# A block's turn and routing logits moved from its first step into its second, ahead of a long hook

## The reference

```
# 1. linear attention with decay: 4 batches, 8 heads, 768 steps, head size 48
cur = einsum(u * k_t, v_t);  y_t = einsum(r_t, state + cur);  state = w * state + einsum(k_t, v_t)
# 2. dense gated layer, d_ff 1536
x = (silu(y @ w_gate) * (y @ w_val)) @ w_out
# 3. mixture of experts: 8 experts, top 1, d_ff 1024
logits = x @ w_gate2; e = argmax(logits); gate = softmax(logits)[e]
eom = 1 / (1 + exp(-(x @ w_output_gate)))
out = gate * eom[e] * (relu(x @ w1[e]) @ w2[e])
```

## Time and profile before

| | |
|---|---|
| median of the runs | 833.06 us (832.24 to 833.59) |
| the profiled execution's own time | 832.38 us |
| its span, first to last instruction | 830.5 us (1.9 us lie around it) |
| TensorE busy, by the profile | 816.4 us, 98% |
| VectorE, ScalarE, GpSimd busy | 58%, 44%, 23% |
| mean granted TensorE clock | 0.998 |

### The profile page before, as it was taken

How to read it: one execution, slowest core, us unless ns; L and a number is a source line. 1 busy time by engine, 2 the same in 40 slices (tenths; PEclk the granted TensorE clock), 3 DMA queues, 4 the chain that set the end, 5 groups by cost and what they waited for, 6 DMA issues and landing times.

```text
span 830.5 us, 19906 instructions
## 1 busy us (share of the span) xinstructions
PE 816.4 (98%) x7813; PEld 719.6 (87%) x7813; DVE 479.3 (58%) x1004; ACT 368.3 (44%) x705; POOL 189.8 (23%) x159
## 2 busy tenths in 40 slices
PE   7999999999999999999999999999999999999996
PEld 4788888888888888888888888899999999999996
DVE  7667743445443535344343453469878977897771
ACT  3635432333323333223332311456566866687661
POOL 3434402322352143404220210004021110111010
PEclk9999999999999999999999999999999999999999
DMA  9445301121211113121100116057997667866700
GB/s 338 160 172 181 118 1 62 62 86 40 97 62 62 39 63 121 63 61 40 63 25 1 40 40 266 2 229 239 353 364 282 246 249 279 303 254 234 286 19 19
DMA packets 24148, 116.72 MB, mean 141 GB/s; under 512 B 3373, under 2 KB 9825, under 8 KB 18449
## 3 DMA queue, kind: packets, MB, share of 16 engines
q1 hardware_dynamic: 19984, 101.16, 33.8%
q0 software_dynamic: 3520, 9.87, 3.1%
q10 hardware_dynamic: 576, 4.72, 1.6%
HBM read 102.64 MB, written 14.16 MB: 141 GB/s over the span
## 4 chain that ended last, share of the span: by engine, by line
PE 98%; DMA 0%; DVE 0%; issue 0%; POOLq 0%; ACT 0%; SPq 0%
PE bank L1775 36%; PE bank L1823 7%; PE bank L1825 6%; PE bank L1824 6%; PE bank L1896 5%; PE bank L1898 5%; PE bank L1897 5%; PE bank L1861 3%; PE bank L1863 3%; PE bank L1862 3%; PE bank L1857 3%; PE bank L1700 2%; PE bank L1650 2%; PE bank L1685 1%; PE bank L1837 1%; PE bank L1858 1%
## 5 line engine op out<-in xcount | busy, mean ns | idle before, releaser
L1355 DVE TENSOR_TENSOR PP<-SG,bank 128x512 f32<-128x512 f32 (+1 forms) x78 | 49.9, 646 | 209.7 <-PE bank L1775 178.0
L1775 PE MATMUL bank<-X1H,WH 128*128 128x512 f32 x432 | 168.7, 391 | 0.0
L1775 PE MATMUL bank<-X1L,WH 128*128 128x512 f32 x432 | 168.0, 390 | 0.2 <-DVE X1L L1179 0.2
L1775 PE MATMUL bank<-X1H,WL 128*128 128x512 f32 x432 | 168.0, 390 | 0.0
L793 ACT ACTIVATE AH<-PP 128x512 fp32r<-128x512 f32 (+1 forms) x78 | 46.0, 597 | 152.7 <-DVE PP L1355 152.7
L897 ACT ACTIVATE SG<-bank 128x512 f32<-128x512 f32 x72 | 43.0, 597 | 158.5 <-PE bank L1775 152.9
L1775 PEld LDWEIGHTS bank<-X1H,WH 128*128 128x128 f32 x432 | 81.0, 188 | 17.9 <-issue 1.0
L1775 PEld LDWEIGHTS bank<-X1H,WL 128*128 128x128 f32 x432 | 81.0, 188 | 17.2 <-DVE WL L1173 0.3
L1775 PEld LDWEIGHTS bank<-X1L,WH 128*128 128x128 f32 x432 | 81.0, 188 | 17.0 <-DVE X1L L1179 0.6
L1823 PE MATMUL bank<-AH,WH 128*128 128x512 f32 (+1 forms) x234 | 91.0, 389 | 0.0
L776 POOL DMA_INDIRECT out<-YO,IDX x31 | 38.5, 1241 | 218.0 <-ACT YO L991 208.5
(11 more groups left out here) (245 smaller groups left out, 1799.7 us busy)
## 6 DMA issues: line engine op xcount, KB each, us to landing
W_EVEN<-w SPq DMA_DIRECT2D x20, 1536.0 KB, 9.1
W_ODD<-w SPq DMA_DIRECT2D x18, 1536.0 KB, 8.7
RK_IN<-unit_rk SPq DMA_DIRECT2D x19, 736.0 KB, 5.3
V_IN<-unit_v SPq DMA_DIRECT2D x20, 480.0 KB, 3.6
STG<-w_dense ACTq DMA_DIRECT2D x4, 1152.0 KB, 5.2
XG_ODD<-store SPq DMA_DIRECT2D x9, 394.0 KB, 8.4
store<-PAD SPq DMA_DIRECT2D x8, 394.0 KB
STG<-w_dense SPq DMA_DIRECT2D x2, 1152.0 KB, 9.4
```

What stands on the lines that cost most here:

```text
L1355: return tt(PP[:, part], SG[:, part], VALUE_PS[:, part], ALU.mult)
L1775: last = mm(bank_[:, :], lhs[:, f, m, k * P:k * P + P], rhs[:, k, :], start=(x == 0), stop=(x == len(terms) - 1))
```

## The change

In blocks 1 to 5 the turn of the rows and the routing logits move from the hook of step 0 to that of step 1. In blocks 1 to 4 the units' hooks move one step earlier, from steps 2, 4, 6, 8 to steps 1, 3, 5, 7, so that turn and logits stand directly ahead of the first long hook. The logits no longer go to the value's bank but to bank 7, columns 384 to 511, beside the scores; so the waits for the value's bank around them go (`value_free` ahead of the logits, `logits_copied` ahead of the value's `up` in step 1), and the scores of a unit now wait for `logits_copied`. The copies that follow the turn and the logits on ScalarE and VectorE move to step 1 as well. In the last block, which has no units, everything of the routing stands one step later: turn and logits in step 1, turned logits in step 2, ranks and positions in step 3. Block 0 keeps its order.

```
     def unit_begun(n, f):
         final = isinstance(n, int) and n >= CH - 2
-        if f in (2, 4, 6) and not (final and n == CH - 1):
+        if isinstance(n, int) and n == 0 and f in (0, 2, 4, 6):
             return units_of_block(n)[f // 2]
-        if f == 0 and isinstance(n, int) and n == 0:
-            return units_of_block(n)[0]
-        if f == 8 and not final:
+        if not (isinstance(n, int) and n in (0, CH - 1)) and f in (1, 3, 5):
+            return units_of_block(n)[f // 2 + 1]
+        if f == (8 if isinstance(n, int) and n == 0 else 7) and not final:
             return units_of_block(n + 1)[0]
         return None
...
-                self.logits = (ps if isinstance(n, int) and n == CH else VALUE_PS)[:, 0:P]
+                self.logits = ps[:, 2 * PART:2 * PART + P]
...
# ScalarE
+                    if f == 1 and not first:
+                        rec_copies(n)
                     begun, ended = unit_begun(n, f), unit_ended(n, f)
...
-                    if f == 0 and not first:
-                        rec_copies(n)
...
# VectorE
-                        if f == 0:
+                        if f == 1:
                             copy_logits(n)
-                        if f == (1 if last else 9):
+                            rec_copy(n)
+                        if f == (2 if last else 9):
                             copy_turned_logits(n)
-                        if f == (2 if last else 10):
+                        if f == (3 if last else 10):
                             copy_ranks(n)
...
-                        if f == 0:
-                            rec_copy(n)
-                        if f == (1 if last else 9):
+                        if f == (2 if last else 9):
                             route(n)
-                        if f == (2 if last else 10):
+                        if f == (3 if last else 10):
                             positions(n)
...
# TensorE
-                    if f == 1 and not first:
-                        pe.wait_ge(logits_copied, n)
...
-                        if f == 0:
+                        if f == 1:
                             turn(n)
-                            pe.wait_ge(value_free, q + 1)
+                            need(pe, ranks_copied, n - 1)
                             route_logits(n)
-                        if f == (1 if last else 9):
+                        if f == (2 if last else 9):
...
-                        if f == (2 if last else 10):
+                        if f == (3 if last else 10):
                             ranks(n)
...
                     if begun:
                         if not begun.in_block_0:
                             pe.wait_ge(silu_ready, q + 1)
+                            need(pe, logits_copied, n)
                             need(pe, ranks_copied, max(n - 1, 0))
                         scores(begun)
```

More of the change, by code:

```diff
@@ L349, in unit_summed @@
     def unit_summed(n, f):
-        if f in (2, 4, 6, 8) and not (isinstance(n, int) and n >= CH - 2):
-            return units_of_block(n)[f // 2 - 1]
+        if isinstance(n, int) and n == 0:
+            return units_of_block(n)[f // 2 - 1] if f in (2, 4, 6, 8) else None
+        if f in (1, 3, 5, 7) and not (isinstance(n, int) and n >= CH - 2):
+            return units_of_block(n)[f // 2]
         return None
     def unit_ended(n, f):
[L357 to L360, removed]
+        if f in (1, 3, 5, 7) and not (isinstance(n, int) and n == CH - 1):
+            return units_of_block(n)[f // 2]
         return None
@@ L1921, in dense_block @@
                     if not first:
-                        if f == 0:
+                        if f == 1:
                             turn(n)
-                            pe.wait_ge(value_free, q + 1)
+                            need(pe, ranks_copied, n - 1)
                             route_logits(n)
-                        if f == (1 if last else 9):
-                            if begun:
-                                pe.wait_ge(parts_masked, 2 * (begun.i - BATCH) + 2)
+                        if f == (2 if last else 9):
+                            if not last and n < CH - 2:
+                                pe.wait_ge(parts_masked, 2 * (units_of_block(n + 1)[0].i - BATCH) + 2)
                             turn_logits(n)
-                        if f == (2 if last else 10):
+                        if f == (3 if last else 10):
                             ranks(n)
```

## The result

| | before | after |
|---|---|---|
| median of 18 runs each, us | 832.78 | 835.77 |
| lowest to highest, us | 831.67 to 834.36 | 834.61 to 841.51 |
| ratio, 95% interval | | 1.0043 (1.0034 to 1.0052) |
| profiled execution, us | 832.38 | 834.61 |
| its span, us | 830.5 | 832.8 |

The change makes the kernel slower, by 0.34% to 0.52%. The forecast was 832.4 us with a range up to 833.6: the sign and the range were both wrong. The profiled execution of after is the fastest of its runs, so what follows accounts for 2.2 us; for the 1.2 us by which the median lies above it no execution was profiled.

What follows compares the result with a forecast made beforehand. TensorE, busy in 98% of the span, was taken as the bound. Four blocks' merge gain of 0.88 us less 0.2 for the new neighbourhood, all else nothing, gave -0.7: 833.06 to 832.4 us, range 831.1 to 833.6.

Steps and rivals of the forecast that it cites:

- Plain steps and the merge: TensorE, blocks 1 to 4: two hooks become one, ups of steps 0 to 2 fall from 12.50 to 12.28 us.
- The charge for the switch: TensorE, blocks 1 to 4: state terms or outputs directly behind the logits cost 0.05 us each, 0.2 us in all.
- The wait that comes. … Cost nothing: Scores of the first long hook wait for `logits_copied`; the copy comes 1.6 us ahead of need, so no cost.
- Last block. … Zero: Last block: turn and logits go from step 0 to 1, hook entry and exit both still paid; no change in time.
- The other half of that step: Last block, VectorE: step 4's product comes 1.5 us late, with 1.5 us of cover, so nobody waits.
- GpSimd: Blocks 2 to 4: RW ready 3.3 us ahead of second unit's scores; rival: late, 839.0 us at most, chance 0.07 with other waits.
- The clock: Dense hooks keep granted clock at 1.00; rival: level lost for a step in four blocks, 24 us, 857, chance 0.01.

Runs made afterwards that it cites:

- e9: After with the last block's turn and logits back in step 0, two repeated score waits dropped, 136 spare waits in block 0: 830.47 us, ratio 0.9983.
- e7: Before with 64 long-met spare waits among the matmuls of block 0's ups, nothing else changed: 835.28 us, ratio 1.0028 to before.
- e8: Before with 128 long-met spare waits among the matmuls of block 0's ups, nothing else changed: 836.44 us, ratio 1.0045 to before.
- e4: After with 128 long-met spare waits among the matmuls of block 0's ups: 834.20 us, ratio 1.0019 to before.
- e6: After with the last block's turn and logits back in step 0, two repeated score waits dropped, 128 spare waits in block 0: 833.39 us, ratio 1.0003.
- e1: After without the scores' repeated waits TensorE had already passed, a spare wait in the following down instead: 835.40 us, ratio 1.0043 to before.
- e2: After with the last block's turn and logits, and what follows them, back in step 0 as in before: 834.60 us, ratio 1.0033 to before.
- e5: After with the last block's turn and logits back in step 0, two repeated score waits dropped, no spare waits: 835.99 us, ratio 1.0030 to before.
- e10: After with the last block's turn and logits back in step 0, two repeated score waits dropped, 212 spare waits in block 0: 832.66 us, ratio 1.0001.
- e11: After with 133 spare waits, its seventh wait and last block left as they are: 833.29 us, ratio 1.0010 to before.

## Why the prediction was wrong

**Plain steps and the merge: right.** 0.22 us a block, as read from the starts. The charge for the switch, 0.05 a block, should have been a gain of 0.11 in blocks 1 to 3. Together e9 against before gives 427.27 - 0.38 - 425.55 = 1.3 us, where 0.7 was forecast and 0.9 the end of the range kept.

**"The wait that comes. … Cost nothing": the step that failed first.** The copy was in time in nine of ten profiles of the new order, as the cover of 1.6 us said. But the wait itself is a part of an instruction of TensorE's, and it stands in every hook with scores, not only in the first one of a block, since the line of the diff is under every unit. In eleven hooks it is the seventh wait and made the fourth semaphore instruction, 0.10 us, 1.1 us in all. Before showed three such instructions at this place; their number and spacing could have been read.

**"Last block. … Zero": failed.** I had carried "the `down` waits for the copies, which end earlier, nothing" from the middle blocks. There 2.9 us of units lie between logits and `down`; in the last block nothing does, and VectorE's copy of the rows, which stands behind its low part and the logits' copy, ends at 480.15, while the `down` could have begun at 479.12. It begins 1.1 us late. The prediction had VectorE's copies as the later ones, and that held. The cover was worked out for one place and used at another. The other half of that step was right: VectorE's product of step 4 begins at 500.77 where the earlier trace rows has 497.29, which is 1.3 us late beside a block that is 2.2 us later, and TensorE waits for nobody there:

```profile
500.77 0.69 DVE L1355 TENSOR_TENSOR PP<-SG,bank 128x512 f32<-128x512 f32 x1
```

**No term for where the instruction pieces end: the largest miss.** A hook that moves a step earlier also moves its instructions by some hundred places in TensorE's stream. Neither sum nor rivals had it. The rows of before that would have hinted at it were there: scores of 1.06 us at 134.03, and a column of instruction packets. It could hardly have been given a sign, only a width. Before has next to no stops by luck, as its shifts show; these versions of one and the same kernel (before, e7, e8) differ by up to 0.45%, 3.7 us, and my whole range was 2.5 us wide.

**GpSimd: right in the likely case.** After the change RW of block 2's second unit ends 3.49 us ahead of its scores, against 3.3 worked out:

```profile
206.31 1.15 POOL L709 TENSOR_TENSOR KH<-RK_IN,POWT 128x448 f32<-128x448 f32 x1 [2.42 <-DMA store<-RC,POSI]
...
211.34 1.28 POOL L704 TENSOR_TENSOR RW_ODD<-RK_IN,POWR 112x512 f32<-112x512 f32 x1
```

**The clock** is at 1.00 in the middle block (203.71 to 293.20), as the earlier trace rows had let expect of dense hooks. It falls behind a long stop (e4, e6), which the hooks themselves don't make.

**What stays open.** Stops come at fixed remainders, but their length does not follow from the place: instruction 7617 cost 0.83 us in after, 1.52 in e1, 0.91 in e2, and nothing in before. It follows from the packet, which took 0.93, 1.32 and 0.92 us in the three; in before it had landed 3.75 us ahead. Why a packet begins late and takes 0.88 to 1.45 us is open. The spread of after's runs (6.9 us against 2.7) fits stops of changing length and the clock behind a long one; no run was profiled at 841.51 to show it. The waits for `XG_ODD` in e5 to e8, and for `HL` in e4, e10 and e11 (0.83 to 1.07 us), are not explained.

## What to carry to other kernels

A wait costs its own instruction even if it is long met: on a queue that is 98% busy count the waits, in every pass that the edited line serves, and drop those the engine has already passed. Work out the cover of a move at each place where the order differs, the last pass above all. And where an engine runs through hundreds of small instructions in a few microseconds, a shift of its stream alone can move the time by half a percent: before a change of that size is believed or dropped, time it, and the old kernel too, with a few different numbers of spare instructions ahead.
